# Output projection of a gated layer: high parts first, and an earlier cast of the next batch's input

## The reference, cut to what matters

```python
h = np.maximum(x @ w_in, 0.0)                      # 768 x 384 @ 384 x 1024
u, v = (h[..., :d_ff // 2], h[..., d_ff // 2:])
mu = np.mean(v, axis=-1, keepdims=True)
var = np.mean((v - mu) ** 2, axis=-1, keepdims=True)
v_n = (v - mu) / np.sqrt(var + 1e-06)
v_s = np.einsum('ts,bsd->btd', w_spatial, v_n) + b_spatial[None, :, None]
gated = u * v_s
return (gated @ w_out).astype(np.float32)          # 768 x 512 @ 512 x 384
```

## Time and profile before

| | |
|---|---|
| median of 3 runs | 739.6 us |
| profiled execution: its own time | 741.86 us |
| profiled execution: span from the first to the last instruction | 740.1 us |
| TensorE matmul busy | 703.6 us (95%) |
| TensorE weight loads busy | 664.0 us (90%) |
| VectorE, ScalarE, GpSimd busy | 395.9, 338.4, 210.5 us |
| mean granted TensorE clock | 1.000 |

### The profile page before, as it was taken

How to read it: one execution, slowest core, us unless ns; L and a number is a source line. 1 busy time by engine, 2 the same in 40 slices (tenths; PEclk the granted TensorE clock), 3 DMA queues, 4 the chain that set the end, 5 groups by cost and what they waited for, 6 DMA issues and landing times.

```text
span 740.1 us, 25675 instructions
## 1 busy us (share of the span) xinstructions
PE 703.6 (95%) x11336; PEld 664.0 (90%) x11336; DVE 395.9 (53%) x668; ACT 338.4 (46%) x573; POOL 210.5 (28%) x141
## 2 busy tenths in 40 slices
PE   2798899999999999999999999999999999999998
PEld 2688789899998899999999899999998998999998
DVE  6888674544664555555553324225933851870671
ACT  5787546435546346446435331334433432532422
POOL 5504480320350220161120231462360060033022
PEclk9999999999999999999999999999999999999999
DMA  9414501211401221311000251002110101101001
GB/s 360 157 46 148 176 4 45 99 57 45 152 4 45 73 83 45 118 37 45 22 18 2 91 150 72 33 11 87 64 40 26 65 12 53 64 0 64 0 0 64
DMA packets 16525, 49.49 MB, mean 67 GB/s; under 512 B 1616, under 2 KB 9552, under 8 KB 15920
## 3 DMA queue, kind: packets, MB, share of 16 engines
q1 hardware_dynamic: 16432, 48.09, 18.5%
HBM read 38.65 MB, written 9.44 MB: 65 GB/s over the span
## 4 chain that ended last, share of the span: by engine, by line
PE 67%; issue 19%; POOL 4%; DVE 3%; ACT 1%; DMA 0%; POOLq 0%; DVEq 0%; ACTq 0%
PE HB L885 23%; PE ZB L962 7%; PE ZB L964 7%; PE ZB L963 7%; PE SB L762 4%; PE ZB L885 3%; PE SB L885 3%; POOL gl L712 3%; PE SB L867 2%; PE SB L876 2%; PE SB L822 2%; POOL x2l L686 1%; PE SB L999 1%; PE SB L837 1%; PE SB L850 1%
## 5 line engine op out<-in xcount | busy, mean ns | idle before, releaser
L1514 DVE SCALAR_TENSOR_TENSOR hid_lo<-HB,hid_hi 128x384 fp32r<-128x384 f32 x96 | 53.3, 556 | 140.9 <-ACT hid_hi L1190 140.1
L1190 ACT ACTIVATE hid_hi<-HB 128x384 fp32r<-128x384 f32 x96 | 47.2, 492 | 158.9 <-PE HB L885 158.7
L885 PE MATMUL HB<-uh,w1h 128*128 128x384 f32 x288 | 103.0, 358 | 4.1 <-DVE ul L1510 1.5
L962 PE MATMUL ZB<-hid_hi,w2h 128*128 128x384 f32 x288 | 98.6, 342 | 0.0
L885 PE MATMUL HB<-ul,w1h 128*128 128x384 f32 x288 | 96.7, 336 | 0.0
L964 PE MATMUL ZB<-hid_lo,w2h 128*128 128x384 f32 x288 | 96.6, 335 | 0.0
L885 PE MATMUL HB<-uh,w1l 128*128 128x384 f32 x288 | 96.5, 335 | 0.0
L963 PE MATMUL ZB<-hid_hi,w2l 128*128 128x384 f32 x288 | 96.3, 334 | 0.0
L1045 ACT COPY Qd<-Q 48x768 f32<-48x768 f32 x84 | 73.0, 870 | 13.6 <-PE SB L762 5.0
L712 POOL TENSOR_TENSOR gl<-gf,gh 128x384 fp32r<-128x384 f32 x32 | 33.2, 1044 | 147.8 <-ACT gh L1230 147.4
L655 POOL TENSOR_TENSOR Q<-Q,bk 112x768 f32<-112x768 f32 x13 | 24.7, 1902 | 174.4 <-ACT Qd L1045 174.4
(11 more groups left out here) (260 smaller groups left out, 1516.4 us busy)
## 6 DMA issues: line engine op xcount, KB each, us to landing
Q<-in_q SPq DMA_DIRECT2D x8, 768.0 KB, 6.0
AL<-in_al SPq DMA_DIRECT2D x7, 768.0 KB, 4.9
K<-in_k SPq DMA_DIRECT2D x7, 768.0 KB, 4.3
Vt<-in_v SPq DMA_DIRECT2D x8, 576.0 KB, 3.9
mid<-x2s SPq DMA_DIRECT2D x8, 576.0 KB, 3.6
x<-mid SPq DMA_DIRECT2D x4, 1152.0 KB, 5.3
out<-o_sb SPq DMA_DIRECT2D x24, 192.0 KB, 1.8
x2s<-in_w SPq DMA_DIRECT2D x9, 384.0 KB, 4.6
```

The source lines that it names most:

```text
L885: last = nc.tensor.matmul(dst, weights(x, w), moving(y, m), start=(n == 0 and x == y == 0), stop=(n == total - 1 and y == 1))
L962: nc.tensor.matmul(bank, w2h[:, i, cols], hi, start=(i == 0), stop=False)
L1190: nc.scalar.activation(hid_hi[:, i % HID, :], HB[i % 2][:, 0:TILE], ACT.Relu).then_inc(h_hi, 1)
L1514: nc.vector.scalar_tensor_tensor(hid_lo[:, i % HID, :], HB[i % 2][:, 0:TILE], 0.0, hid_hi[:, i % HID, :].bitcast(F32), ALU.max, ALU.subtra ...
```

## The change

Two edits. In an `o` group TensorE no longer goes through `split_product`: it first waits for the high parts (`gh_done`) and issues the eight matmuls with `gh` as weights, by `woh` and `wol` in turn, and then waits for `gl_done`, at the same count, and issues the four matmuls with `gl`. And ScalarE casts the next batch's x2 behind its work for P5, f = 1, instead of P7, f = 1.

```diff
+X2_GROUP = ("s", "P5", FP - 1)
...
                     pe.wait_ge(wo_lo, 1)
-                    pe.wait_ge(gl_done, NHALF * FGB * b + (NHALF * FGB if i < HS else 3 * FP))
-                    last = split_product(bank[:, 0:DM],
-                                         lambda x, f: (gh, gl)[x][:, f, i * P:(i + 1) * P],
-                                         lambda y, f: (woh, wol)[y][:, f, :], [(f, f) for f in range(FGB)], FGB)
+                    rows = slice(i * P, (i + 1) * P)
+                    gates = NHALF * FGB * b + (NHALF * FGB if i < HS else 3 * FP)
+                    pe.wait_ge(gh_done, gates)
+                    for f in range(FGB):
+                        for w in (woh, wol):
+                            nc.tensor.matmul(bank[:, 0:DM], gh[:, f, rows], w[:, f, :], start=(f == 0 and w is woh),
+                                             stop=False, skip_group_check=True)
+
+                    pe.wait_ge(gl_done, gates)
+                    for f in range(FGB):
+                        last = nc.tensor.matmul(bank[:, 0:DM], gl[:, f, rows], woh[:, f, :], start=False,
+                                                stop=(f == FGB - 1), skip_group_check=True)
...
             for j in range(TWO.n):
                 two_group(0, j, True)
-                if TWO.groups[j][:3] == ("s", "P7", 1):
+                if TWO.groups[j][:3] == X2_GROUP:
                     x2_high(1, False)
             with act.Fori(1, BATCH - 1) as b:
                 for j in range(TWO.n):
                     two_group(b, j, False)
-                    if TWO.groups[j][:3] == ("s", "P7", 1):
+                    if TWO.groups[j][:3] == X2_GROUP:
                         x2_high(b + 1, False)
```

## The result

The changed kernel takes 735.47 us, the median of 10 runs (734.24 to 739.88); the kernel before 739.1 us over the 10 runs beside it (738.21 to 743.63). The ratio is 0.9949, 95% interval 0.9932 to 0.9967. That is 3.6 us less, where 3.45 were forecast, and 735.5 us against a forecast of 736.2. It is within 1%, as forecast. The interval of the ratio stands for a gain of 2.4 to 5.0 us, so the times alone show that there is a gain, and the profiles must show that it is this one.

A forecast was written before the change was run, and what follows sets the result against it. TensorE's stream was taken as the bound, with stalls of 1.02, 1.15, 1.15 and 0.13 us waiting for `gl`. Removing all 3.45 us, with new waits at 0, took 739.6 to 736.2 us; range 734.5 to 740.8.

The forecast's parts named there:

- Only TensorE's stream counts, and stage two has one stall: TensorE busy 703.6 of 740.1 us; from 497 us on it waits only for GpSimd's `gl`, costing 3.45 us.
- The stall is the sixth `gl`, late because of the casts of x2: First output group, batches 0 to 2: ScalarE's 2.30 us of casts delay P3's gates, so `gl` ends at 604.93 (batch 1).
- The move alone would leave 0.5 us: Casts moved behind P5 without the split: about 0.13 us left in each batch, 0.5 of 3.45 us.
- The split alone would do it all, with 0.3 us to spare: Output groups split, casts unmoved: whole 3.45 us gone, sixth `gl` at 604.93 against 605.26.
- The new waits cost 0: Middle wait in 24 output groups: taken as 0, upper bound 4.5 us at 0.188 us each.
- rival 3: Each new middle wait in the output groups bares a weight load, up to 4.5 us in all: 740.7 us; chance 0.06.
- The casts cost nothing in their new place: ScalarE between P2's and P7's gates: casts end at 595.64, P7's first gate starts at 597.62, 1.98 us slack.
- GpSimd beside VectorE: P3's first `gl` beside VectorE's second P3 gate: even 0.48 us of disturbance leaves `gh` 0.64 us early, so 0.
- The rival of the late load (4): x2 lands late, so P7's casts queue behind its casts on ScalarE: at most 743.9 us; chance 0.02.
- The median: Whole-kernel forecast for the median of the runs: 739.6 less 3.45 gives 736.2 us, 0.47% less.

The follow-up runs named there:

- the doubled kernel: Kernel before with the three casts of x2 done twice in batches 0 to 2, still behind P7: 750.29 us, ratio 1.0123.

## Why the prediction was right, step by step

- *Only TensorE's stream counts, and stage two has one stall.* Right. The stall was 3.45 us, and stage two became 3.45 us shorter. Reading its size from the second matmul instead of from the idle times mattered: the wait list had 2.6 us.
- *The stall is the sixth `gl`, late because of the casts of x2.* Right, and shown both ways. Taken off the stretch in either direction (behind P5 or P3) the casts leave 0.10 to 0.15 us; doubled in place they add 2.3 to 2.5 us of waiting for each batch.
- *The move alone would leave 0.5 us.* 0.52 was left (0.10 + 0.14 + 0.13 + 0.15).
- *The split alone would do it all, with 0.3 us to spare.* 239.63 us against 239.62, with 0.33 to spare. So the two edits overlap: the move alone takes 2.94 of the 3.45 us and the split alone 3.44. What the move adds to the split is no time but margin, 1.42 us instead of 0.33 at the ninth matmul.
- *The new waits cost 0.* Right: 240 more of them change stage two by -0.07 us. One argument around it was wrong. The prediction cites the Trainium skill (TensorE: Matmul & The Clock Gate, Part 3, "The mechanism") for a rule that a weight load overlaps a matmul in flight only where their row groups differ, and says that by this rule the 4.5 us of rival 3 would be certain. It does not follow: a load that can never hide is bare in both kernels, which have the same loads, and the difference would be 0. The rule does not hold for this stream of full-height matmuls either: loads of 0.188 us go on at 0.17 us from start to start with a wait ahead of each. The same section of the Trainium skill also lets a load run ahead where it goes to a background weight buffer, and the prediction left that out; the pace agrees with it, but no run here shows where a load goes. The forecast did not rest on it, but what was said for rival 3 was weaker than it looked.
- *The casts cost nothing in their new place.* Right, with 2.07 us of idle time behind them where 1.98 was expected. Even doubled they cost nothing.
- *GpSimd beside VectorE.* The second P3 gate, which now runs beside a `gl`, kept its 0.56 us: the sixth `gh` had 1.13 us to spare where 1.12 was expected.
- *The rival of the late load (4)* was not met. The load can hold the casts back, and does so by 2.33 us when they stand behind P1.
- *The median.* 736.2 was 739.6 - 3.45. The median before fell to 739.1 with more runs, which accounts for 0.5 of the 0.7 us between forecast and result; the other 0.2 is well inside the scatter of the runs. That the medians differ by nearly the 3.45 is in part luck, as their interval is 2.4 to 5.0; stage two in the profiles, 3.45 shorter, is what bears the size out.

## What to carry to other kernels

Where an engine's queue mixes work that someone waits for with work that no one does yet, look at the slack behind each place: the same 2.3 us was free in one gap and cost 1.0 to 1.15 us in the next. A product in high and low parts can start on the part that is made first, if each part has a wait of its own; here such a wait cost nothing when it was satisfied, and some 0.24 us when it had to block briefly. Measure each of two edits alone: here the split gave all of the time, and the move nothing beside it but margin. And when two profiles are compared, set them side by side by stage: here half of the difference in span lay where nothing had been changed.

## What the runs showed that was not expected

A stall can cost more than its length. Around waits of 3.1 and 3.2 us TensorE worked at half its clock, 1.2 of 2.4 GHz, for 5.4 us in one batch and 3.5 us in another, 4.0 us lost, and not at all after a wait of 3.2 us in the batch between them. After the waits of 0.8 to 1.6 us in the kernel before and in the split one with doubled casts, the clock stayed at 1.00 in stage two. In the profile of the doubled kernel the half clock made the loss by waiting (7.15 us) more than half as large again. Its four runs lie between 747.96 and 753.48 us; whether the clock is behind that scatter is not shown, since both the fastest and the slowest have a mean clock of 0.98 over the whole run. The Trainium skill (TensorE: Matmul & The Clock Gate, Part 1, "What's actually happening") tells of these two levels and of a free-running window, which does not start with the kernel. By that, equal waits may fall differently on the window; the three batches agree with it, and no run here tests it.
